# Moving expert 0's low weight parts and a weight load behind the routing, with another order of the attention rounds

## The chip, the cores and the metric

The kernel runs on one core of a Trainium2 chip. The metric is the device time of one execution in microseconds. The core has five engines with a queue each: TensorE (PE, matmuls; its weight loads are listed as PEld), VectorE (DVE), ScalarE (ACT), GpSimd (POOL) and SyncE (SP, which here only issues transfers). Each runs its own list of instructions in order, and they wait for each other by semaphores. Transfers run on 16 DMA engines; SP, ACT and POOL issue them.

## The reference

Three stages in a row, all in float32:

```
attention, for each batch (2) and head (8), state 48 x 48, 768 steps:
    y[t]  = r[t] @ (state + outer(u * k[t], v[t]))
    state = w * state + outer(k[t], v[t])
mixture of experts, on x = y with heads side by side (384 wide), 8 experts:
    fresh = argmax(x @ w_gate);  gate = sigmoid(x @ w_local)
    e[s]  = fresh[s] if s == 0 or gate[s] < 0.5 else e[s-1]
    out   = softmax(x @ w_gate)[e] * (relu(x @ w1[e]) @ w2[e])
last layer:  out = x + relu(norm(x) * g @ w_ch1) @ w_ch2
```

The expert of a token can be that of the token before it, so the choice is a scan along the sequence. The weights are w1 384 x 1024 and w2 1024 x 384 for each expert, and 384 x 1536 and 1536 x 384 for the last layer.

## The kernel before

**Attention.** The 1536 tokens are 12 chunks of 128 (NT = 12, the two batches in turn). A loop of rounds i = 0 to 13 runs on every engine, each with its own part. In round i PE makes the scores of chunk i (L1128), transposes the finished X rows of chunk i-2 (L1135), multiplies the state (L1147) and the masked scores (L1153) for chunk i-1, makes the router's logits of chunk i-2 (L1166), the state's update (L1177), and turns y back (L1184). DVE adds the diagonal term into X for chunk i-2 (L836), masks the scores (L846), sums the state (L853), scales the keys of chunk i+1 (L825) and makes the diagonal (L863, L865). ACT copies the transposed X for the router (L620), multiplies the diagonal by v, four heads before and four behind its copy of y (L609, L629), and copies the logits to LG (L632). POOL makes the products r * k (L535), the scaled r and k (L525, L544) and the decayed state (L552).

**Routing** is done in two phases: chunks 0 to 7 while the last rounds still run, and chunks 8 to 11 behind them. In each: `choose` (DVE, L762 to L771) takes the argmax and makes a code, `code_rows` (PE) turns the codes into a row, `carry_on` (DVE, L777 and L778) makes a mask of tokens that keep the expert of the one before and scans, `expert_columns` (PE) turns back, `chosen` (DVE) makes the one-hot and the gate weight, `counts` (PE) sums over tokens, and `places` (DVE, L808 to L818) gives each token its row in a buffer `xsort` in memory, sorted by expert. POOL then scatters the rows of one chunk with each indirect transfer (L518), eight for phase 0 and four for phase 1. From the counts DVE makes a small integer table `meta` (L879 to L900); each engine then loads loop bounds from it, one count at a time (`expert_regs`, L310; on SP L447 and L448).

**Weights.** Matmuls are made nearly exact by splitting each weight into a high and a low part. ACT makes the high part (`split_hi`, L359), DVE and POOL the low part by a subtraction (`split_lo`, L364), in 6 pieces of 128x1024 for each expert: POOL the first two, DVE the other four. For expert 0 this is done inside the attention rounds: ACT in rounds 6 to 11, POOL in 10 and 11, DVE in 9, 11, 12 and 13 (`LATE_LO`). There are two raw buffers. The weights of expert 2 go where those of expert 0 were; SP loads them when expert 0's are split (L417, L418, run as L342 and L344). For later experts ACT loads those of e+2 at the start of expert e's first tile.

**Experts.** Tokens of one expert are taken in tiles of 256. The first tile's rows come by one load when all scatters have landed (L433). PE transposes them (L1199), ACT and DVE round them (L654, L910), and PE multiplies, three matmuls for one product (L1204 to L1206). The rows of later tiles go by SP into a ring in X (L443), then by POOL's copy (L569) to where PE transposes them, in the middle of the tile before. PE waits at the start of each expert for all of its split pieces (`split_done`).

Of the kernel before, what the change touches and what calls it, by code (L numbers as in the profile page):

```python
# [28 lines left out]
P = 128  # L29
# [5 lines left out]
def program(nc, rkT, rows_kr, rows_v, w, u, w_small, wexp, wch, gain_in, out, xsort, ysort, dims):  # L35
# [30 lines left out]
    with ctx:  # L66
# [55 lines left out]
        M_TILES, M_BEFORE, M_ROWS, M_ENDS, M_GROUP = (i * E for i in range(5))  # L122
        M_BEHIND = M_GROUP + NG
        M_MORE = M_BEHIND + 1
        meta = sb("meta", [1, M_MORE + 1], I32)

# [125 lines left out]
        s_row = sem("code_row_made")  # L252
        s_er = sem("expert_row_made")
# [44 lines left out]
        ROUTED = (NT - 2, NT + 1)  # L298
        HALF_WEIGHTS = (2, 4, 6, 8)
        LATE_LO = (NT - 3, NT - 1, NT, NT + 1)  # L300
        def need(eng, s, n):
            if n > 0:
                eng.wait_ge(s, n)

        def expert_regs(eng, offsets=False):
# [8 lines left out]
            rows = [eng.value_load(meta[0:1, M_ROWS + e:M_ROWS + e + 1], min_val=0, max_val=TOK)  # L314
                    for e in range(E)] if offsets else None
            behind = eng.value_load(meta[0:1, M_BEHIND:M_BEHIND + 1], min_val=0, max_val=NT + E)
            more = eng.value_load(meta[0:1, M_MORE:M_MORE + 1], min_val=0, max_val=NT)
            return tiles, before, rows, behind, more
# [61 lines left out]
        def _(sp):  # L380
# [36 lines left out]
            split_done(sp, 0)  # L417
            load_weights(sp, 2)  # L418

# [14 lines left out]
            sp.wait_ge(s_meta, 1)  # L434

# [9 lines left out]

            for e in range(E):
                tiles = sp.value_load(meta[0:1, M_TILES + e:M_TILES + e + 1], min_val=1, max_val=NT)  # L447
                before = sp.value_load(meta[0:1, M_BEFORE + e:M_BEFORE + e + 1], min_val=0, max_val=NT + E)  # L448
                with sp.Fori(0, tiles) as i:
                    load_rows(before + i, nc.s_assert_within(  # L450
                        i * MT + e * CAP, e * CAP, e * CAP + TOK,
                        skip_runtime_bounds_check_because="an expert's tiles begin before its rows end"))
# [3 lines left out]
            groups = [sp.value_load(meta[0:1, M_GROUP + g:M_GROUP + g + 1], min_val=1, max_val=NT + E)  # L456
                      for g in range(NG)]
# [10 lines left out]
        def _(pool):  # L468
# [60 lines left out]
            for i in range(NT + 2):  # L529
# [25 lines left out]
                if NT - B <= i < NT:  # L555
                    split_lo(pool, 0, i - NT + B)
            assert B == POOL_CK

            for ph in range(NPH):
                scatter(ph)  # L560
# [168 lines left out]
        def _(dve):  # L729
# [101 lines left out]
            for i in range(NT + 2):  # L831
# [16 lines left out]
                if i == ROUTED[0] + 2:  # L848
                    places(0)
# [496 lines left out]
```

## Time and profile before

| | us |
|---|---|
| median of 3 runs | 416.61 (416.61, 416.61, 418.36) |
| the profiled execution | 418.34 |
| its span, first to last instruction | 416.7 |
| PE busy in the span | 375.9 (90%) |
| DVE, ACT, POOL busy | 218.6, 146.6, 138.4 |

Times in the rows are counted from the start of the span. [...]

### The profile page before, as it was taken

The numbers are of one execution on the slowest core, as the hardware profiler recorded it, in microseconds if no ns is written. First come the engines' busy times: TensorE is split into PE (matmuls) and PEld (weight loads), VectorE is DVE, ScalarE is ACT, GpSimd is POOL, SyncE is SP. The second block draws the span as 40 slices with busy tenths as digits, with TensorE's granted clock in tenths as the row PEclk, the third lists the DMA queues.
The fourth block names the chain that finished last, engine by engine and source line by source line (L and its number), as shares of the span: only waits on it lengthen the run. The fifth ranks groups of instructions, "written<-read, shape, count | busy, mean of one in ns | idle before, by whom it ended". The sixth has DMA issues, their size and how long they took to land.

```text
span 416.7 us, 7567 instructions
## 1 busy us (share of the span) xinstructions
PE 375.9 (90%) x2768; PEld 347.8 (83%) x2768; DVE 218.6 (52%) x412; ACT 146.6 (35%) x295; POOL 138.4 (33%) x134
## 2 busy tenths in 40 slices
PE   6799998660299999999999998999999999999993
PEld 5688886550299999999999997889998899988993
DVE  5687779846036647366482798675213651133110
ACT  0355676520053725438264471632002220023000
POOL 5989777384050532605235040400110000100010
PEclk9699999855589999999999999999999999999998
DMA  6989980049446774948627340600110001100000
GB/s 204 327 324 400 371 295 2 0 161 386 140 152 205 294 283 149 375 160 328 252 90 265 106 164 2 191 0 2 38 39 0 1 2 38 39 0 2 19 24 35
DMA packets 17018, 61.07 MB, mean 147 GB/s; under 512 B 2128, under 2 KB 9808, under 8 KB 14672
## 3 DMA queue, kind: packets, MB, share of 16 engines
q1 hardware_dynamic: 12240, 25.87, 17.8%
q10 hardware_dynamic: 2304, 26.74, 17.4%
q0 software_dynamic: 2432, 7.92, 5.0%
q8 instruction: 24, 0.39, 0.4%
q14 instruction: 18, 0.15, 0.1%
HBM read 49.42 MB, written 11.10 MB: 145 GB/s over the span
## 4 chain that ended last, share of the span: by engine, by line
PE 79%; DVE 8%; DMA 4%; POOL 4%; issue 3%; ACT 1%; SPq 1%; DVEq 0%; ACTq 0%; POOLq 0%
PE bank L1204 22%; PE bank L1206 22%; PE bank L1205 22%; POOL xsort L518 3%; PE bank L1128 3%; PE bank L1147 2%; PE bank L1153 2%; DMA tin<-in_rkT 2%; PE bank L1199 1%; DVE split L364 1%; PE bank L1166 1%; DMA xsort<-X,cpos 1%; PE bank L1135 1%; PE bank L1184 1%; PE bank L1177 1%
## 5 line engine op out<-in xcount | busy, mean ns | idle before, releaser
L359 ACT CAST split<-raw 128x1024 fp32r<-128x1024 f32 (+1 forms) x60 | 59.2, 1005 | 0.0
L1204 PE MATMUL bank<-xT,split 128*128 128x256 f32 x192 | 55.2, 288 | 2.1 <-DVE xT L910 2.1
L599 POOL DMA_INDIRECT out<-orow,cpos x12 | 11.6, 970 | 132.7 <-DVE orow L1039 132.7
L1205 PE MATMUL bank<-xT,split 128*128 128x256 f32 x192 | 55.0, 286 | 0.0
L1206 PE MATMUL bank<-xT,split 128*128 128x256 f32 x192 | 55.0, 286 | 0.0
L364 DVE TENSOR_TENSOR split<-raw,split 128x1024 fp32r<-128x1024 f32 (+1 forms) x40 | 51.2, 1294 | 1.9 <-ACT split L359 1.7
L1204 PE MATMUL bank<-split,h2T 128*128 128x384 f32 x144 | 48.7, 338 | 0.0
L1206 PE MATMUL bank<-split,h2T 128*128 128x384 f32 x144 | 48.2, 335 | 0.0
L1205 PE MATMUL bank<-split,h2T 128*128 128x384 f32 x144 | 48.2, 335 | 0.0
L364 POOL TENSOR_TENSOR split<-raw,split 128x1024 fp32r<-128x1024 f32 (+1 forms) x20 | 45.7, 2304 | 6.3 <-ACT split L359 6.2
L718 ACT ACTIVATE h2T<-bank 128x512 fp32r<-128x512 f32 x36 | 21.5, 598 | 72.8 <-PE bank L1206 71.7
L1051 DVE SCALAR_TENSOR_TENSOR h2T<-bank,h2T 128x512 fp32r<-128x512 f32 x36 | 24.9, 691 | 37.5 <-ACT h2T L718 37.4
L1204 PE MATMUL bank<-split,hT 128*128 128x384 f32 x128 | 43.7, 341 | 0.0
L1204 PE MATMUL bank<-split 128*128 128x512 f32 x108 | 42.1, 390 | 1.2 <-DVE split L942 1.2
L1206 PE MATMUL bank<-split,hT 128*128 128x384 f32 x128 | 42.8, 335 | 0.0
L676 ACT ACTIVATE hT<-bank 128x512 fp32r<-128x512 f32 x32 | 19.1, 597 | 67.4 <-PE bank L1206 67.4
L1205 PE MATMUL bank<-split,hT 128*128 128x384 f32 x128 | 42.8, 334 | 0.0
L1206 PE MATMUL bank<-split 128*128 128x512 f32 x108 | 42.1, 389 | 0.0
L1205 PE MATMUL bank<-split 128*128 128x512 f32 x108 | 42.1, 389 | 0.0
L958 DVE SCALAR_TENSOR_TENSOR hT<-bank,hT 128x512 fp32r<-128x512 f32 x32 | 22.0, 687 | 36.6 <-ACT hT L676 36.6
L1204 PEld LDWEIGHTS bank<-xT,split 128*128 128x128 f32 x192 | 37.6, 196 | 2.5 <-DVE xT L910 2.5
L1205 PEld LDWEIGHTS bank<-xT,split 128*128 128x128 f32 x192 | 37.6, 196 | 0.0
(161 smaller groups left out, 698.9 us busy)
## 6 DMA issues: line engine op xcount, KB each, us to landing
raw<-in_wexp ACTq DMA_DIRECT2D x14, 1536.0 KB, 9.4
tin<-in_rkT SPq DMA_DIRECT2D x12, 512.0 KB, 7.7
kr<-in_rows_kr SPq DMA_DIRECT2D x12, 384.0 KB, 6.2
raw<-in_wch ACTq DMA_DIRECT2D x2, 2304.0 KB, 9.6
xsort<-zeros SPq DMA_DIRECT2D x8, 388.0 KB, 5.3
X<-xsort SPq DMA_DIRECT2D x8, 388.0 KB, 5.9
ysort<-yrow POOLq DMA_DIRECT2D x8, 388.0 KB, 7.3
raw<-in_wexp SPq DMA_DIRECT2D x2, 1536.0 KB, 9.5
```

The lines of the kernel that those rows point to most:

```text
L359: act.copy(hi, src).then_inc(s_hi, 1)
L364: eng.tensor_tensor(lo, src, hi.bitcast(F32), ALU.subtract).then_inc(s_lop if c < POOL_CK else s_lod, 1)
L518: pool.indirect_dma_start(out=xsort, out_offset=bass.IndirectOffsetOnAxis(ap=cpos[:, j:j + 1], axis=0), in_=X[:, j, :], in_offset=None).th ...
L599: pool.indirect_dma_start(out=out, out_offset=bass.IndirectOffsetOnAxis(ap=cpos[:, j:j + 1], axis=0), in_=orow[j % 2][:, :], in_offset=Non ...
L676: act.activation(hT[:, 0, x * FU:(x + 1) * FU, :], bank[HB[x]][:].rearrange("p (f t) -> p f t", f=FU), ACT.Relu).then_inc(m_h, 1)
L718: act.activation(h2T[:, f, 0, :], bank[HB2[f % 3]][:], ACT.Relu).then_inc(f_ra, 1)
L958: dve.scalar_tensor_tensor(out=hT[:, 1, q, :].rearrange("p f t -> p (f t)"), in0=bank[HB[x]][:], scalar=0.0, in1=hT[:, 0, q, :].rearrange( ...
L1051: dve.scalar_tensor_tensor(out=h2T[:, f, 1, :], in0=bank[HB2[f % 3]][:], scalar=0.0, in1=h2T[:, f, 0, :].bitcast(F32), op0=ALU.max, op1=AL ...
L1128: last = pe.matmul(bank[2 + h][:, n * P:(n + 1) * P], kT[b][q, n, :], rT[i % 3][q, n, :], start=True, stop=True)
L1204: pe.matmul(dst, stationary[0], moving[0], start=first, stop=False)
L1205: pe.matmul(dst, stationary[0], moving[1], start=False, stop=False)
L1206: return pe.matmul(dst, stationary[1], moving[0], start=False, stop=last)
```

## The change

Five edits. The low parts of expert 0's weights leave the rounds: POOL makes its two behind the last scatter, DVE its four behind `meta`; ACT makes the high parts one round earlier (5 to 10). The load of expert 2's weights leaves SP and is done by ACT at expert 0's first tile. In a round DVE masks the scores behind the state's sum and the keys' scaling, and ACT multiplies all eight heads by the diagonal ahead of its copy for the router. In the routing of phase 0 the steps move: `choose` to the end of round 10, `code_rows` and `carry_on` to round 11, `expert_columns` to the start of round 12, `counts` to the start of round 13, `places` behind the rounds; the mask `keep` of phase 0 is made by ACT as relu(1 - code), into a new semaphore. The exponentials of phase 0 move from round 10 to 11. And each engine loads the counts that it needs in one or two instructions in place of one for each.

```diff
-        ROUTED = (NT - 2, NT + 1)
-        LATE_LO = (NT - 3, NT - 1, NT, NT + 1)
+        ROUTED = NT - 2
+        def load_many(eng, a, b, most):
+            return nc.values_load_multi_w_load_instructions(
+                meta[0:1, a:b], engines=(eng.engine,), min_val=0, max_val=most, ...)[1]
@@ expert_regs
-            tiles = [eng.value_load(meta[0:1, M_TILES + e:M_TILES + e + 1], min_val=1, max_val=NT) for e in range(E)]
+            said = load_many(eng, M_TILES, M_BEHIND + 1, NT + E)
...
+            rows = load_many(eng, M_ROWS, M_ROWS + E, TOK) if offsets else None
@@ SP
-            split_done(sp, 0)
-            load_weights(sp, 2)
...
-            sp.wait_ge(s_meta, 1)
             sp.sem_inc(m_in, 16)
...
+            tiles, before, _, _, _ = expert_regs(sp)
             for e in range(E):
-                tiles = sp.value_load(meta[0:1, M_TILES + e:M_TILES + e + 1], min_val=1, max_val=NT)
-                before = sp.value_load(meta[0:1, M_BEFORE + e:M_BEFORE + e + 1], min_val=0, max_val=NT + E)
@@ POOL
-                if NT - B <= i < NT:
-                    split_lo(pool, 0, i - NT + B)
             for ph in range(NPH):
                 scatter(ph)
+            for c in range(POOL_CK):
+                split_lo(pool, 0, c)
@@ ACT
-                if i >= 2:
-                    act.wait_ge(s_xt, i - 1)
-                    act.copy(xTa[:], bank[7][:, 0:D]).then_inc(s_xc, 1)
...
-                    dg_times_v(j, range(H // 2))
+                    dg_times_v(j).then_inc(s_dvp, 1)
+                if i >= 2:
+                    act.wait_ge(s_xt, i - 1)
+                    act.copy(xTa[:], bank[7][:, 0:D]).then_inc(s_xc, 1)
...
-                if NT - CK <= i < NT:
-                    split_hi(act, 0, i - NT + CK)
+                if NT - CK - 1 <= i < NT - 1:
+                    split_hi(act, 0, i - NT + CK + 1)
+                if i == ROUTED + 1:
+                    act.wait_ge(s_row, 1)
+                    n = PHASES[0][1] // B * P
+                    act.activation(keep[:, 0:n], bank[6][0:B, 0:n], ACT.Relu, bias=goes_on[0][0:B, 0, 1:2], scale=-1.0).then_inc(s_keep, 1)
+                    exps(0)
+            exps(1)
...
-                    if starts and e > 0:
+                    if starts:
                         split_done(act, e)
                         load_weights(act, e + 2)
@@ DVE
@@ carry_on
+                if ph == 0:
+                    dve.wait_ge(s_keep, 1)
+                else:
+                    link(dve.tensor_scalar(keep[:, a:b], bank[6][0:B, 0:b - a], 0.0, None, ALU.is_equal))
@@ the rounds: in round i now X, stsum, scale_k(i + 1), masks sc, rku, dg, and then
-                if i == ROUTED[0]:
+                if i == ROUTED:
+                    dve.wait_ge(s_late, 1)
+                    choose(0)
+                if i == ROUTED + 1:
                     carry_on(0)
-                if i == ROUTED[0] + 1:
+                if i == ROUTED + 2:
                     chosen(0)
-                if i in LATE_LO:
-                    split_lo(dve, 0, POOL_CK + LATE_LO.index(i))
+            places(0)
...
+            for c in range(POOL_CK, CK):
+                split_lo(dve, 0, c)
             dve.sem_inc(m_y, XR)
@@ PE
+                if i == ROUTED + 2:
+                    expert_columns(0)
+                if i == ROUTED + 3:
+                    counts(0)
                 if i >= 2:
                     pe.wait_ge(s_x, i - 1)
...
-                if i == ROUTED[0] + 2:
-                    counts(0)
...
-                if i == ROUTED[0]:
+                if i == ROUTED + 1:
                     pe.wait_ge(s_late, 1)
                     code_rows(0)
-                if i == ROUTED[0] + 1:
-                    expert_columns(0)
```

## Rows read from the trace of the kernel before

**Rows 1.** The chain that ended last, by engine (the page).

```profile
PE 79%; DVE 8%; DMA 4%; POOL 4%; issue 3%; ACT 1%; SPq 1%; DVEq 0%; ACTq 0%; POOLq 0%
```

**Rows 2.** Stretches: length, busy of PE, PEld, DVE, ACT, POOL, PEclk, DMA, GB/s.

```profile
64.01:69.60 5.59, 5.59 (x80) 4.68 (x80) 5.45 (x14) 3.66 (x12) 3.05 (x3) 1.00 0.00 0
...
80.50:113.20 32.70, 11.78 (x69) 9.07 (x69) 13.65 (x61) 4.78 (x16) 13.59 (x12) 0.50 0.62 219
113.20:116.80 3.60, 3.60 (x17) 3.60 (x18) 0.00 (x0) 0.00 (x0) 0.00 (x0) 0.50 0.18 32
```

**Rows 3.** The chain in order of time: start, us, what.

```profile
101.56 4.91 DMA xsort<-X,cpos
106.53 2.98 DMA xrow<-xsort
```

**Rows 4.** Timeline of POOL, scatters 1, 4, 9, 12: start, us, engine, what, [idle before].

```profile
83.51 2.08 POOL L518 DMA_INDIRECT xsort<-X,cpos  x1 [5.95 <-DVEq L819]
...
88.42 1.91 POOL L518 DMA_INDIRECT xsort<-X,cpos  x1 [0.30 <-issue]
...
97.77 0.96 POOL L518 DMA_INDIRECT xsort<-X,cpos  x1 [2.37 <-DVEq L819]
...
101.56 0.96 POOL L518 DMA_INDIRECT xsort<-X,cpos  x1 [0.30 <-issue]
```

**Rows 5.** Timeline of ACT in round 9.

```profile
60.15 0.48 ACT L620 COPY xTa<-bank 128x384 f32<-128x384 f32 x1 [0.75 <-PE bank L1135]
60.52 1.01 ACT L609 ACTIVATE dv<-vn,dg 128x48 f32<-128x48 f32 x4
```

**Rows 6.** Timeline of DVE beside the scatters.

```profile
83.31 1.23 DVE L364 TENSOR_TENSOR split<-raw,split 128x1024 fp32r<-128x1024 f32 x1
...
88.28 1.22 DVE L364 TENSOR_TENSOR split<-raw,split 128x1024 fp32r<-128x1024 f32 x1
...
97.27 0.17 DVE L818 CAST cpos<-ec 128x4 int32<-128x4 f32 x1
...
101.61 0.14 DVE L896 CAST meta<-cnt 1x1 int32<-1x1 f32 x1
```

**Rows 7.** Timeline, one POOL and one DVE product side by side, and the latter alone.

```profile
61.31 0.97 POOL L552 TENSOR_TENSOR state<-stsum,wst 128x192 f32<-128x192 f32 x1 [1.10 <-DVE stsum L853]
61.75 0.95 DVE L863 TENSOR_TENSOR rku<-rk,ub 128x384 f32<-128x384 f32 x1
...
74.25 0.55 DVE L863 TENSOR_TENSOR rku<-rk,ub 128x384 f32<-128x384 f32 x1
```

**Rows 8.** Timeline of PE and DVE from round 11 on, the waits of the routing.

```profile
70.90 1.21 DVE L778 TENSOR_TENSOR_SCAN er<-keep,bank 2x512 bf16<-2x512 f32 x1
...
72.94 0.55 PE L1135 MATMUL bank<-ident,X 128*128 128x128 f32 x3 [1.85 <-DVE X L836]
...
80.46 0.90 PE L1135 MATMUL bank<-ident,X 128*128 128x128 f32 x3 [3.52 <-DVE X L836]
...
87.81 0.56 DVE L836 TENSOR_TENSOR X<-bank,dv 128x384 f32<-128x384 f32 x1 [3.27 <-ACT dv L609]
...
91.58 0.18 DVE L762 TENSOR_REDUCE mx<-LG 128x4 f32<-128x32 f32 x1 [2.08 <-ACT LG L632]
```

**Rows 9.** DMA issues near 86, 115 and 151.7: KB each, median us to landing.

```profile
xsort<-X,cpos POOLq DMA_INDIRECT x2, 3.3
...
X<-xsort SPq DMA_DIRECT2D x1, 388.0 KB, 3.3
...
X<-xsort SPq DMA_DIRECT2D x1, 388.0 KB, 8.4
```

**Rows 10.** Timeline of POOL and PE, tile 2's rows in the first tile.

```profile
118.63 0.83 POOL L569 COPY xrow<-X 128x768 f32 x1 [16.11 <-DMA X<-xsort]
...
123.52 0.82 PE L1199 MATMUL bank<-ident,xrow 128*128 128x128 f32 x6
```

**Rows 11.** SP's loads of single counts: duration ns min/median/max.

```profile
L447 SPq TENSOR_LOAD <-meta x8: 262/266/275, 107.0 to 179.0; - x8
```

More of the change, by code:

```diff
@@ L118, in program @@
         cnt_i = sb("cnt_i", [1, 2, E], I32)
[L122 to L125, printed above, removed]
+        M_TILES, M_MORE, M_BEHIND, M_GROUP = 0, E, E + 1, E + 2
+        M_ROWS, M_ENDS = 2 * E, 3 * E
+        assert M_GROUP + NG <= M_ROWS
+        meta = sb("meta", [1, M_ENDS + E], I32)
         gcol = sb("gcol", [P, KD])
@@ L303, in need @@
                 eng.wait_ge(s, n)
+        def load_many(eng, a, b, most):
+            return nc.values_load_multi_w_load_instructions(
+                meta[0:1, a:b], engines=(eng.engine,), min_val=0, max_val=most,
+                skip_runtime_bounds_check_because="counts of rows that there are, and of their tiles")[1]
         def expert_regs(eng, offsets=False):
             eng.wait_ge(s_meta, 1)
-            tiles = [eng.value_load(meta[0:1, M_TILES + e:M_TILES + e + 1], min_val=1, max_val=NT) for e in range(E)]
+            said = load_many(eng, M_TILES, M_BEHIND + 1, NT + E)
+            tiles = [nc.s_assert_within(said[e], 1, NT, skip_runtime_bounds_check_because="counts rounded up to tiles, "
+                                        "at least one") for e in range(E)]
+            more = nc.s_assert_within(said[M_MORE], 0, NT, skip_runtime_bounds_check_because="one less than a number of tiles")
             before = [0]
@@ L313, in expert_regs @@
                 before.append(eng.snap(before[e] + tiles[e], min_val=0, max_val=NT + E))
[L314 to L318, printed above, removed]
+            rows = load_many(eng, M_ROWS, M_ROWS + E, TOK) if offsets else None
+            return tiles, before, rows, said[M_BEHIND], more
         def over_tiles(eng, e, tiles, more, tile):
@@ L444, in load_rows @@
                              xsort[bass.ds(start, MT), :].rearrange("(h p) d -> p h d", p=P)).then_inc(m_in, 16)
+            tiles, before, _, _, _ = expert_regs(sp)
             for e in range(E):
[L447 to L450 removed]
+                with sp.Fori(0, tiles[e]) as i:
+                    load_rows(before[e] + i, nc.s_assert_within(
                         i * MT + e * CAP, e * CAP, e * CAP + TOK,
@@ L455, in _ @@
                     sp.wait_ge(s_fill, 16 * (e + 2))
-            groups = [sp.value_load(meta[0:1, M_GROUP + g:M_GROUP + g + 1], min_val=1, max_val=NT + E)
-                      for g in range(NG)]
+            groups = [nc.s_assert_within(x, 1, NT + E, skip_runtime_bounds_check_because="a group's rows are of one expert at least")
+                      for x in load_many(sp, M_GROUP, M_GROUP + NG, NT + E)]
             for g in range(NG):
@@ L605, in _, with dg_times_v, exps @@
         def _(act):
-            def dg_times_v(j, heads):
+            def dg_times_v(j):
                 b = j % B
-                for h in heads:
+                for h in range(H):
                     last = act.activation(dv[b][:, h, :], vn[j % VRING][:, h, :], ACT.Copy, scale=dg[b][:, h:h + 1])
                 return last
+            def exps(ph):
+                act.wait_ge(s_sub, ph + 1)
+                act.activation(pe_[:, slice(*PHASES[ph])], le[:, slice(*PHASES[ph])], ACT.Exp).then_inc(s_exp, 1)
             for i in range(NT + 2):
@@ L857, in _ @@
                 if i < NT:
+                    b = i % B
+                    dve.wait_ge(s_scp, i + 1)
+                    need(dve, s_yp, i - B + 1)
+                    for h in range(2):
+                        dve.tensor_tensor(sc[b][:, h], bank[2 + h][:].rearrange("p (n t) -> p n t", n=NP),
+                                          causal[:].unsqueeze(1).broadcast_to([P, NP, P]), ALU.mult).then_inc(s_sc, 1)
                     dve.wait_ge(s_rk, i + 1)
```

26 lines of the change are left out of this document (3 added, 23 removed).

## The prediction

> **What bounds the kernel.** I read the chain of waits by engine first [rows 1]: TensorE (PE) carries 79% of the span, so a change beside PE pays only where PE waits. The table by stage says where that is [rows 2]: an attention round in full swing (64.0 to 69.6) keeps PE busy for all of its 5.59 us at the full clock, while from 80.5 to 113.2 it works 11.8 of 32.7 us, at half clock. Last I read what ends that gap [rows 3]: the last of 12 row scatters (issued at 101.56, landed 4.91 us later at 106.47), then the load of the sorted rows (2.98 us), then 6.65 us of transposes, register work and rounding to the first expert product at 113.2. Everything before the change's stage is bound by PE, everything behind 113.2 by PE too; the change lives in the stretch between 64 and 113, and there the chain is: places of phase 0, eight scatters, places of phase 1, four scatters, landing. The scatters themselves leave every 1.27 us (97.77 to 101.56 is three of them) [rows 4].
>
> **The parts.**
>
> *Attention rounds.* VectorE (DVE) does the state sum and the key scaling ahead of the masks, ScalarE (ACT) does all eight diagonal products ahead of the copy for the router. Nothing is added, and PE fills the whole round [rows 2], so I cost it at nothing. What hides it: ACT waits 0.75 us for PE before its copy, and four diagonal products take it 1.01 [rows 5]; the second four now stand in front too, so the copy comes about 0.3 late, and PE reads it only behind two groups of 16 matmuls. If the diagonal came late, every round would pay (a rival below).
>
> *The low parts leave rounds 9 to 13.* DVE gives up four subtractions of 1.23 us [rows 6] and GpSimd (POOL) two. DVE and POOL also block each other: POOL's state product at 61.31 takes 0.97, the DVE product begun meanwhile at 61.75 takes 0.95, and the same product with POOL quiet at 74.25 takes 0.55 [rows 7]. So the X additions of rounds 11 and 12, for which PE waited 1.85 and 3.52 us [rows 8], come earlier. But on that same path the change puts the carry mask on ACT, behind its logits copy. Step by step: round 11 starts on PE at 69.6; scores, transposes, both products and the code row end at about 73.5; ACT is free for the mask only behind PE's logits, 74.5, and needs about 0.6; DVE's scan takes 1.21 [rows 8], so the expert row is there at 76.3. PE stands still from 74.9 to 76.4, now in front of round 12. Round 12 has 45 of round 10's 80 matmuls, the longer ones, about 3.7 us at full clock, plus 0.6 for the ACT copy in its middle: 81.0. Before, the counts were done 0.9 us after 80.46 and the places 1.9 us later (a subtraction starts behind them at 83.31) [rows 6, 8]. Now counts at 81.2, the last X addition to 81.5, places done at 83.2. **The first scatter stays at 83.5.** That is my main reading: phase 0 gains nothing, because its counts and places now stand behind round 12's work.
>
> *Phase 1 comes 8 us earlier.* Its first instruction waited for the last logits until 91.58, held up by half-clock PE work, a 3.27 us wait of DVE for the diagonal products at 87.81, and one more subtraction [rows 8]. Now the logits follow the X addition at 81.5 by about 2.1 us: 83.6. Its own work took 5.86 us (91.58 to 97.44) [rows 6, 8], so its places are ready at 89.5 and the counts table (4.3 us, 97.44 to 101.75) at 93.8. Before, POOL had run dry for 2.37 us in front of scatter 9 [rows 4], of which 0.3 is the usual gap. That 2.07 us goes: the 12 scatters now run in one row. What is late next is POOL's issuing itself.
>
> *The subtractions land on the scatters.* Scatters 1 and 4 took 2.08 and 1.91 us against 0.96 for the others, and each starts within 0.2 us of a DVE subtraction (83.31, 88.28) [rows 4, 6]: each waited until that ended. DVE now runs its four subtractions from 93.8 to 98.4, on top of scatters 9 to 12. If POOL slips in between two of them, as its state product did [rows 7], each hit scatter waits about 1.0 and its successor starts inside the next but one subtraction: two are hit, 2.0 us, the same as the 2.07 lost before. If none is hit: 0. If POOL stays shut out for all four: 4.6. I take 2.0. The sum for the last scatter's issue: 83.5 + 11 x 1.27 + 2.0 = 99.5, against 101.56: 2.1 us earlier. POOL's two own subtractions then end at about 105.2 and the first product needs them at about 109: hidden, with 4 us to spare.
>
> [...] The rows show long scatters beside a DVE tensor-tensor subtraction [rows 4, 6]. [...]
>
> *The third weight load leaves the window.* Two transfers of 1536 KB started at 89.6; scatters that were issued before them landed after 3.3 us, the last one, in their wake, after 4.91 [rows 3, 9]. With nothing beside it I take 3.0, as the rows' own load took [rows 3]; the ends are 3.3, and 2.7 if half a neighbour's issue was in that: 1.9 us earlier. It is issued now by ACT at the start of the first expert tile (about 112.3 in the old times). Price there: a row load without weights beside it lands in 3.3 us, with them in 8.4 [rows 9]. The rows of tile 2 would land near 121 to 122.5 and POOL's 0.83 us copy end at 122 to 123.4, against 119.5 before; PE reads them at 123.52 [rows 10]. So the cover shrinks from 4 us to about nothing. POOL's subtractions for expert 1 slip 3 us behind the copy and push DVE's. I take 0.6 us of PE waiting at the first tile and its border, from 0 to 3.
>
> *One load for the counts.* On SyncE (SP) a count costs a 0.27 us load and about 0.3 of checks [rows 11]; two per expert go, ten in one instruction come once, between 0.3 and 2.7 us, behind the issue of the first row load, and hide or cost under the previous point. I take 0. On the other engines the loads ran in the wait for the rows, and they start 8 us earlier now.
>
> *Clock.* PE restarts cold behind the gap either way: 3.6 us at half clock behind 113.2 [rows 2], which cost 1.8. Another such stretch may come out longer or not; I take 0.3, from 0 to 1.8.
>
> **Sum**: 2.1 + 1.9 - 0.6 - 0.3 = 3.1 us faster. The profiled execution took 418.34 (416.7 of span, 1.6 around it), which is 1.7 above the median; the difference carries over: 415.2 for an execution like that one, **413.5** for the median.
>
> **Rivals.**
> [...]
> - *POOL is shut out by four subtractions in a row*: last issue at 102.0, 2.6 later than forecast, 416.1. Against: [rows 7].
> - *PE falls to half clock in front of round 12.* It fell before in the 3.52 us wait and did not in the 1.85 us one [rows 2, 8]; the new wait is 1.5 plus a short one behind it. If it falls, the 3.7 us of round 12 take 3 more, all places come 3 us later, last issue 102.5: 416.5.
> - *Slower: the router's copy misses PE in every round.* ACT's eight diagonal products (two times 1.01 us) need the diagonal, which DVE now makes behind the masks, and both stand in front of the copy. In the old times PE wants the copy about 7.5 us after the previous masks begin. It decides where the diagonal is ready more than 1.2 us later than I reckon (DVE held by POOL's key product in each round). At 0.7 a round over ten rounds: 7.0 - 3.1 slower, 420.5. For: DVE and POOL hold each other up already. Against: PE's full round, and DVE's idle share.
> - That the change does nothing can be only if the end of the gap is set elsewhere; the chain [rows 3] leaves no other.
>
> **Numbers.** Forecast 0.55, no hold-up 0.12, shut out 0.11, half clock 0.12, slower 0.10. Half a per cent, 2.1 us, is about what can be told from no change: faster means under 414.5. Of the forecast's 0.55 about 0.47 lies below that, with 0.12 from the first rival: faster 0.59; same 0.31 (0.08 + 0.11 + 0.12); slower 0.10. The forecast's own range is 411.8 to 415.3; for 8 in 10 it must hold the two cases near 416 and most of the first rival: 411.0 to 417.0.
>
> **What would show it.** Right: first scatter near 83.5, no gap in front of the ninth, the last issued near 99.5 and landing in about 3; scatters 9 to 12 alternately 0.96 and 2; first expert product near 109.2; a PE wait below 1 us in the first tile. Wrong: PE waits inside rounds 3 to 9; half clock before 82; a first scatter beyond 85; all four last scatters long; a wait of more than 2 us for the rows of the second tile.

## The result, and the profile after

The changed kernel took 419.0 us (median of 20 runs, 416.6 to 421.51), the kernel before, run beside it, 417.99 (20 runs, 416.19 to 418.92): a ratio of 1.0042, 95% interval 1.0026 to 1.0057. It is 0.4% slower. 413.5 was forecast, 411.0 to 417.0 the range, so the time lies outside it. Part of the distance is the base: 413.5 was counted down from a median of three runs, 416.61, and the median of 20 is 417.99; from that one the same sum gives 414.9. Ratios here leave out runs more than 1.5% above the fastest of their kernel: three of 12 with the load issued later, one of 12 with the start repaired, and none of the others. The profiled execution took 421.01 with a span of 419.2, at the upper end of its runs; the one of before had 416.7. The two traces differ by 2.5 us of span, and the rows say where.

The chain by engine has hardly changed its shape [rows 1]; this is its line:

```profile
PE 80%; DMA 6%; DVE 5%; issue 3%; POOL 3%; SPq 1%; ACT 1%; POOLq 0%; DVEq 0%
```

The table by stretches of the kernel after (window, us of it, then busy time of PE, PEld, DVE, ACT and POOL, the granted clock PEclk as a share of full speed, the DMA share, GB/s) answers to [rows 2]:

```profile
64.84:70.39 5.55, 5.55 (x79) 4.64 (x78) 4.97 (x14) 3.88 (x14) 1.93 (x2) 1.00 0.00 0
75.50:77.50 2.00, 0.35 (x6) 0.16 (x4) 1.43 (x3) 2.00 (x9) 0.00 (x0) 1.00 0.00 0
77.50:78.00 0.50, 0.01 (x1) 0.00 (x0) 0.50 (x2) 0.34 (x2) 0.00 (x0) 0.54 0.00 0
78.00:83.00 5.00, 4.97 (x37) 3.82 (x38) 1.33 (x9) 0.75 (x2) 0.00 (x0) 0.50 0.00 0
...
113.41:118.00 4.59, 4.59 (x21) 4.59 (x22) 0.00 (x0) 0.34 (x1) 0.00 (x0) 0.50 0.79 284
118.00:118.50 0.50, 0.50 (x5) 0.50 (x4) 0.21 (x1) 0.50 (x2) 0.00 (x0) 0.50 0.95 399
118.50:119.00 0.50, 0.50 (x6) 0.50 (x6) 0.48 (x1) 0.50 (x1) 0.00 (x0) 1.00 1.03 434
```

A round in full swing is as full as before. The third column from the right, the clock, matters here: PE works 0.35 of the 2 us up to 77.5, the clock falls to half, and round 12, in which PE does not stand still (4.97 of 5.00 us), runs at half clock. Behind the gap the half clock lasts from 113.41 to 118.5, 5.1 us, where it was 3.6 [rows 2].

The timeline of the same kernel (start, us, engine, line, operation, count, and in brackets the idle time before it and what ended that) shows the waits of the routing, the scatters and the first tile, against [rows 4], [rows 6], [rows 8] and [rows 10]:

```profile
75.22 0.67 ACT L640 ACTIVATE keep<-bank,goes_on 2x512 f32<-2x512 f32 x1
...
76.00 1.21 DVE L783 TENSOR_TENSOR_SCAN er<-keep,bank 2x512 bf16<-2x512 f32 x1 [2.07 <-ACT keep L640]
...
77.27 0.25 PE L1096 MATMUL bank<-identb,er 2*128 2x2 bf16 x4 [1.65 <-DVE er L783]
78.03 0.90 PE L1140 MATMUL bank<-ident,X 128*128 128x128 f32 x3 [0.52 <-DVE X L841]
...
85.05 0.56 DVE L841 TENSOR_TENSOR X<-bank,dv 128x384 f32<-128x384 f32 x1 [5.58 <-PE bank L1185]
...
87.52 1.19 POOL L517 DMA_INDIRECT xsort<-X,cpos  x1 [15.53 <-DVEq L824]
...
88.82 0.19 DVE L764 TENSOR_REDUCE mx<-LG 128x4 f32<-128x32 f32 x1 [1.65 <-ACT LG L634]
...
97.86 0.96 POOL L517 DMA_INDIRECT xsort<-X,cpos  x1 [0.30 <-issue]
...
99.10 4.68 DVE L369 TENSOR_TENSOR split<-raw,split 128x1024 fp32r<-128x1024 f32 x4
...
100.39 1.96 POOL L517 DMA_INDIRECT xsort<-X,cpos  x1 [0.30 <-issue]
102.65 1.96 POOL L517 DMA_INDIRECT xsort<-X,cpos  x1 [0.30 <-issue]
104.63 4.64 POOL L369 TENSOR_TENSOR split<-raw,split 128x1024 fp32r<-128x1024 f32 x2
...
124.81 1.08 POOL L566 COPY xrow<-X 128x768 f32 x1 [15.54 <-DMA X<-xsort]
...
125.95 0.77 PE L1200 MATMUL bank<-ident,xrow 128*128 128x128 f32 x5 [1.41 <-POOL xrow L566]
```

PE's waits of 1.85 and 3.52 us for the X additions [rows 8] have become one of 1.65 and one of 0.52, in front of round 12. What follows is long: round 12 keeps PE from 78.0 to 85.0, DVE stands idle for 5.58 us until its last X addition, and the first scatter is at 87.52 instead of 83.51. Of these 4.0 us 0.8 are older than round 12: rounds 2 to 10 all begin that much later than before (round 2 at 20.52 instead of 19.67, round 10 at 64.84 instead of 64.01). Phase 1's choice begins at 88.82 instead of 91.58, and the gap of 2.37 us in front of the ninth scatter [rows 4] is gone; the last is issued at 102.65, 1.1 later than before, of which two held-up scatters make 2.0.

The chain in order of time (start, us, what), against [rows 3] and the loads of [rows 9]:

```profile
102.65 4.02 DMA xsort<-X,cpos
106.75 0.38 SPq L435
...
114.73 9.67 DMA X<-xsort
124.84 1.06 POOL xrow L566
125.95 0.88 PE bank L1200 x6
```

The last scatter takes 4.02 us from issue to landing, 1.0 of it the hold-up, so about 3.0 with no weights beside it. The first product starts at 113.41, against 113.18 before: the later scatter and the quicker landing cancel. Then the load of the second tile's rows takes 9.67 us, and PE stands for 1.41 us in the middle of the first tile. From the start of the first tile to that of the second, 21.57 us pass instead of 19.34: those 2.2 us, and the 0.2 in front, are the whole difference of the traces.

Each run also records its span and mean granted clock. The 20 runs of the kernel after lie between (span 414.4, clock 0.954) and (419.8, 0.939), six of them at 0.938 or 0.939 with spans of 419.1 to 419.8, the profiled one among them. So the share of half clock is not the same in every run; what it costs is what the experiments had to give.

### The profile page after: what moved, and what is told of

Read it like the earlier page. It is cut to its first block, busy times and chain, and to the rows that moved or that the text cites. A ratio compares the mean times of both kernels' runs of the same rounds, so it can differ in the third digit from the quotient of the medians.

```text
span 419.2 us, 7375 instructions
## 1 busy us (share of the span) xinstructions
PE 377.9 (90%) x2768; PEld 349.8 (83%) x2768; DVE 216.0 (52%) x410; ACT 146.6 (35%) x296; POOL 136.4 (33%) x134
## 4 chain that ended last, share of the span: by engine, by line
PE 80%; DMA 6%; DVE 5%; issue 3%; POOL 3%; SPq 1%; ACT 1%; POOLq 0%; DVEq 0%
PE bank L1205 21%; PE bank L1206 21%; PE bank L1207 21%; PE bank L1156 3%; PE bank L1150 3%; PE bank L1129 3%; POOL xsort L517 2%; DMA X<-xsort 2%; PE bank L1167 2%; PE bank L1185 2%; DMA tin<-in_rkT 2%; PE bank L1140 1%; PE bank L1178 1%; PE bank L1200 1%; DMA xsort<-X,cpos 1%
## 5 line engine op out<-in xcount | busy, mean ns | idle before, releaser
L369 DVE TENSOR_TENSOR split<-raw,split 128x1024 fp32r<-128x1024 f32 (+1 forms) x40 | 52.8, 1340 | 2.1 <-ACT split L364 1.9
```

The costliest lines, as they stand in the source:

```text
L369: eng.tensor_tensor(lo, src, hi.bitcast(F32), ALU.subtract).then_inc(s_lop if c < POOL_CK else s_lod, 1)
```

## The experiments

Four theories stood against each other, and the text below calls them by these names. The clock theory: the clock that falls in the wait in front of round 12 costs what was forecast as gain. The load theory: the third weight load (that of expert 2) costs more at the first tile than it gives at the last landing. The order theory: the reordered rounds cost something that I had put at nothing. The scatter theory: the low parts on the scatters cost more than the old gap. The A and B in the recorded expectations are those of each run alone. Ratios below are to runs of the kernel before taken beside them, with the 95% interval. The filler products write to a PSUM bank that nobody reads and take nothing out of the computation.

**PE kept busy in the wait** (the kernel after, with fillers):

```diff
+                     keep_busy(24)
                      expert_columns(0)
+                     keep_busy(8)
```

`keep_busy(n)` makes n products of 128x128 in bf16; both calls stand at the start of round 12.

> The changed kernel, with 24 small matmuls on an unused PSUM bank ahead of TensorE's wait for the expert row in round 12 and 8 behind the expert columns. Theory A (the clock falls to half in the gap between 75.6 and 78.0, and round 12 pays for it): the granted clock stays 1.00 through round 12, the first scatter goes from 87.5 to 84 to 84.7, the last one leaves about 3 us earlier, and the time falls by 2.5 to 3.5 us against the changed kernel (ratio to before 0.995 to 0.998). Rival B (the first scatter is late for the order of the steps, not the clock): first scatter stays above 86.5, time unchanged at 1.004.

Measured: 415.84 us (6 runs, 415.29 to 416.71), 0.9948 (0.9932 to 0.9964), against 1.0042 without: 0.9% by the ratios, 3.2 us by the medians, for a row of products that nobody uses. The table by stretches and the timeline:

```profile
75.60:78.00 2.40, 2.09 (x35) 1.76 (x33) 2.05 (x5) 2.09 (x10) 0.00 (x0) 1.00 0.00 0
78.00:83.00 5.00, 4.39 (x50) 3.47 (x50) 2.33 (x13) 1.23 (x3) 0.00 (x0) 1.00 0.01 3
```

```profile
77.88 0.55 PE L1146 MATMUL bank<-ident,X 128*128 128x128 f32 x3
...
82.43 0.55 PE L1146 MATMUL bank<-ident,X 128*128 128x128 f32 x3 [0.59 <-DVE X L841]
...
84.30 1.18 POOL L517 DMA_INDIRECT xsort<-X,cpos  x1 [12.47 <-DVEq L824]
```

The clock stays at full up to 83.0, round 12 takes 3.9 us (77.88 to 81.8), the first scatter is at 84.30 (forecast 83.5), the last at 99.99 (99.5), the first product at 109.39 (109.2). The clock theory holds, and with the clock kept, the forecast's sum for the gap holds nearly step by step. What is left of the forecast's shortfall is behind 109: here too PE waits 1.41 us for the second tile's rows.

**The same fillers in the kernel before**, in its two waits:

```diff
+                 if i in (NT - 1, NT):
+                     keep_busy(24 if i < NT else 56)
```

> The kernel before, with filler matmuls in its two waits for X: 24 in round 11, 56 in round 12. Theory A (the clock's fall is a loss of both kernels; in the kernel before it delays phase 1, not the first scatter): clock 1.00 through round 12, first scatter unchanged near 83.5, phase 1's places 2 to 3 us earlier, so GpSimd's gap in front of scatter 9 closes and the time falls by 1.5 to 2.1 us, ratio 0.995 to 0.997. Rival B (the kernel before gains nothing since GpSimd's issuing bounds it): 1.000.

Measured: 415.95 us (12 runs), 0.9954 (0.9937 to 0.9971). The old order gained too: the ninth scatter came at 93.84, with its gap down to 0.62, and the last at 97.63, 3.9 us earlier than before. Of these 0.8 stood there from round 2 on (18.83 instead of 19.67), and the first tile gave 1.05 back (20.39 us instead of 19.34, with 6.2 us at half clock behind the gap instead of 3.6), so the span is 2.1 shorter. So with the clock held on both sides the change is worth 0.06%, nothing. The clock explains why it came out slower; it does not by itself explain why it isn't 3 us faster.

**The third weight load alone** (the kernel before, this one part done):

```diff
-             split_done(sp, 0)
-             load_weights(sp, 2)
...
-                     if starts and e > 0:
+                     if starts:
```

> The kernel before, with nothing changed but the load of expert 2's weights: no longer by SyncE when expert 0's parts are split, but by ScalarE at the first tile. Theory A: the last scatter lands 3.0 us after its issue in place of 4.9 (1.9 gained) and the second tile's rows land in 8 to 10 us in place of 3.3 (2.0 to 2.5 lost in the first tile): net between 0 and 1 us slower, ratio 1.000 to 1.003. Rival B (the load costs nothing at the tile, the loss of the changed kernel comes from its late low parts): 1.5 to 2 us faster, 0.995 to 0.997.

Measured: 417.49 us (12 runs), 0.999 (0.9974 to 1.0005). Its chain:

```profile
101.81 2.64 DMA xsort<-X,cpos
...
113.19 9.45 DMA X<-xsort
```

and PE's timeline, the first tile's transposes and the second's:

```profile
108.92 1.54 PE L1197 MATMUL bank<-ident,xrow 128*128 128x128 f32 x6 [13.34 <-issue]
...
124.84 0.88 PE L1197 MATMUL bank<-ident,xrow 128*128 128x128 f32 x6 [1.41 <-POOL xrow L567]
```

The last scatter lands after 2.64 us instead of 4.91 [rows 3]: what the prediction gained there, 1.9, is there, and 0.4 more. But only 0.6 of it reaches the first product (112.55 against 113.18). The first tile's rows, whose load was issued at 104.52 and took 3.0, lay ready at 107.5, and PE began at 108.92, released by "issue": by nothing that the profile shows. The program has only PE's register work on the counts in this place (here still the single loads), so that is the likely cause; no run has this load moved and the counts in one load, and nothing else. Then the row load of tile 2 takes 9.45 us, PE waits 1.41 for it, and the first tile takes 21.33, 2.0 more. In the timed runs gain and loss cancel. The load theory holds in the form that the part is worth nothing, and the trace shows an interplay that the prediction lacked: this part needs the counts earlier or loaded faster to be worth its 2 us in front of the first product. In the kernel after they are both, and its row load is followed by the first product after 6.66 us, as before, not 8.03.

**The load issued later** (the kernel after; expert 2's weights issued behind the rounding of the second tile's rows):

```diff
-                         load_weights(act, e + 2)
+                         if e > 0:
+                             load_weights(act, e + 2)
...
+                         if starts and e == 0:
+                             load_weights(act, 2)
```

> The changed kernel, with the load of expert 2's weights issued by ScalarE behind the rounding of the second tile's rows (about 12 us later) in place of at the start of the first tile. Theory A (the second tile's rows stand behind the weights in the DMA engines: landing 9.7 us after issue, TensorE waits for them in the first tile): the row load lands in 3 to 4 us, the wait of about 2.4 us in the first tile goes, and the kernel is 2.0 to 2.5 us faster than the changed one, so about level with the kernel before (ratio 0.998 to 1.000). Rival B (the row load is slow for another reason, the fill of zeros or the four-row prefetch): landing stays over 8 us and the time stays where the changed kernel's is, 1.004.

Measured: 417.58 us (12 runs, 414.07 to 421.44), 0.9973 (0.9941 to 1.0004). By the means of all runs this kernel is level with the one before (417.69 against 417.72) and 1.6 us under the one after (419.25). The DMA issues from 109 to 140 us (operation, count, KB each, median us to landing):

```profile
raw<-in_wexp ACTq DMA_DIRECT2D x4, 1536.0 KB, 12.4
X<-xsort SPq DMA_DIRECT2D x4, 388.0 KB, 3.3
```

The row loads land in 3.3 us again, PE waits for none of them, and the first tile takes 19.85 instead of 21.57. The weights' own 12.4 us are hidden. The wide interval is the clock again: three of these runs have 0.938 or 0.939, at 420.4 to 421.4, four 0.956 or more, at 414.1 to 414.9.

**Both repairs** (fillers and late load):

> The changed kernel with both repairs: the filler matmuls before and behind the expert columns in round 12, and expert 2's weights loaded behind the rounding of the second tile's rows. Theory A (clock and weight load are two separate losses of the changed kernel, about 3 and 2.2 us, and add up): 5 to 6 us faster than the changed kernel, 413 to 414, ratio to before 0.989 to 0.992, all runs within 2 us of each other. Rival B (one of them hides the other): no better than with the filler alone, 0.995.

Measured: 415.53 us, 0.9944 (0.9923 to 0.9964). That is the rival's figure: only 0.3 us under the fillers alone, where 1.4 was to be had. The trace names the rest: no wait for rows, but behind the gap the half clock lasted till 115.9, 6.2 us, and the first tile took 20.44; and round 2 began at 21.34, where the kernel before has 19.67. That second number pointed at the order theory.

**The start of the rounds** (the kernel after; in round 0 alone the masks stand ahead of the next round's key scaling, as before the change):

```diff
-                 if i + 1 < NT:
-                     scale_k(i + 1)
-                 if i < NT:
+                 def masks():
...
+                 if i == 0:
+                     masks()
+                 if i + 1 < NT:
+                     scale_k(i + 1)
```

> The changed kernel with one edit: in round 0 VectorE masks the scores before it scales the keys of round 1. Theory A (the new order costs about 1 us at the start, once, and every later round is shifted by it): round 2 starts at 19.0 to 19.9 in place of 20.2 to 21.3, the time falls by 0.7 to 1.5 us against the changed kernel, ratio to before 1.000 to 1.003. Rival B (the start shifts with the arrival of the transfers): ratio stays 1.004 and round 2 starts beyond 20.2.

Measured: 417.59 us (12 runs, 414.18 to 422.12), 1.0 (0.9971 to 1.0029), against 1.0042 (1.0026 to 1.0057). The timelines of the kernel after and of this one, in that order:

```profile
13.41 2.08 PE L1129 MATMUL bank<-rT,kT 64*128 64x128 f32 x16 [4.26 <-DVE sc L855]
...
10.28 1.78 DVE L830 TENSOR_TENSOR kT<-tin,wn 128x512 f32<-128x512 f32 x1 [2.42 <-DMA tin<-in_rkT]
11.99 1.28 DVE L855 TENSOR_TENSOR sc<-bank,causal 128x512 f32<-128x512 f32 x2
```

```profile
9.27 1.29 DVE L853 TENSOR_TENSOR sc<-bank,causal 128x512 f32<-128x512 f32 x2 [0.84 <-PE bank L1135]
10.48 1.74 DVE L830 TENSOR_TENSOR kT<-tin,wn 128x512 f32<-128x512 f32 x1
...
12.32 1.16 PE L1135 MATMUL bank<-rT,kT 64*128 64x128 f32 x16 [3.16 <-DVE kT L830]
```

In round 0 the key scaling waits 2.42 us for a transfer (`tin<-in_rkT`). In the changed order the masks queue behind it and PE's next scores wait for them (4.26 us). With the masks first they are done in that wait, and the scores start 1.1 us earlier, at 12.32. Once the rounds are in swing the two orders are equal: 5.54 us from round 2 to 3 and from there on, in both (20.52 to 26.06 and 18.12 to 23.66). All traces together say the same: round 1's scores start at 13.41 to 14.30 in the six with the changed order, at 12.49 to 13.14 in the four with the old one, and at 11.86 to 13.20 in the four with the masks first in round 0. The order theory holds, as a cost of the first rounds alone, about 1.1 us, and not in the form of the prediction's slower rival.

Two things in this pair are not the edit's. Round 2 starts 2.4 us earlier, not 1.1, since the clock, which fell at 13.9 here and at 12.7 in the kernel after, was back at 17.3 here and at 19.5 there. Such a stretch of half clock in round 1 lasted 3.4 us in four of the 14 traces and 6.8 in ten; the short ones are three of the four with the masks first, one of the four with the old order and none of the six with the changed one, and no run shows whether the order has a part in that. And in round 12 of this trace, which has no fillers, the clock fell as well, but came back in the middle of the round:

```profile
75.00:77.50 2.50, 1.98 (x17) 1.54 (x16) 1.92 (x10) 0.93 (x3) 0.00 (x0) 0.56 0.00 0
77.50:83.00 5.50, 4.34 (x44) 3.40 (x40) 1.86 (x8) 1.23 (x3) 0.00 (x0) 0.89 0.01 3
```

It was at half from 75.3 to 78.7. So of the 4.1 us by which the first scatter is earlier (83.44 against 87.52), the new start has 2.4 and the clock in round 12 the rest.

**The start and both repairs together:**

> As the kernel with both repairs, and VectorE masks the scores of round 0 before it scales the keys of round 1, as the kernel before does; all later rounds keep the new order. Theory A (in round 0 the masks stand behind the keys' transfer, and TensorE's second scores wait for them, which delays every round by about 0.5 us): the second scores start at 13.0 to 13.2 in place of 13.4 to 14.3, and the time falls by 0.3 to 0.8 us. Rival B (the later start comes from when the transfers arrive): no difference.

Measured: 413.6 us (412.73 to 414.92), 0.9912 (0.989 to 0.9935): 1.9 us between its median and that of both repairs alone, 0.3% by the ratios. 0.3 to 0.8 us was forecast. Rounds 1 and 2 begin at 11.86 and 17.88 instead of 14.24 and 21.34, and all of these 3.46 us are still there at the first scatter, 81.82 against 85.28. Here too a part is the clock's: in round 1 it was at half for 3.4 us instead of 6.8.

**The carry mask back on DVE** (both repairs, 16 fillers in place of 24):

```diff
-                     act.activation(keep[:, 0:n], bank[6][0:B, 0:n], ACT.Relu, bias=goes_on[0][0:B, 0, 1:2], scale=-1.0)...
...
+                 link(dve.tensor_scalar(keep[:, a:b], bank[6][0:B, 0:b - a], 0.0, None, ALU.is_equal))
```

> As the kernel with both repairs, but the mask of phase 0 is made by VectorE from the code row, as in the kernel before, with 16 filler matmuls in place of 24 since the gap is shorter. Theory A (the mask on ScalarE waits behind its logits copy and costs 0.8 to 1.0 us on the path to the expert row): expert row 0.8 to 1.0 us earlier, first scatter and total earlier by 0.7 to 0.9 us. Rival B (the last X addition and round 12 hide it): no difference in the total.

Measured: 414.23 us (413.52 to 414.91), 0.9925 (0.9906 to 0.9944), against 0.9944 (0.9923 to 0.9964) for both repairs alone. Its timeline, and then that of the kernel with ACT's mask:

```profile
74.90 0.68 DVE L779 TENSOR_SCALAR keep<-bank 2x512 f32<-2x512 f32 x1 [0.46 <-PE bank L1084]
75.62 1.21 DVE L780 TENSOR_TENSOR_SCAN er<-keep,bank 2x512 bf16<-2x512 f32 x1
```

```profile
75.99 0.17 ACT L634 COPY LG<-bank 128x9 f32<-128x9 f32 x1 [0.48 <-PE bank L1176]
76.06 0.67 ACT L640 ACTIVATE keep<-bank,goes_on 2x512 f32<-2x512 f32 x1
...
76.83 1.21 DVE L786 TENSOR_TENSOR_SCAN er<-keep,bank 2x512 bf16<-2x512 f32 x1 [2.06 <-ACT keep L640]
```

The same mask takes 0.68 us on DVE, which stood idle at that point, and 0.67 on ACT, where it queues behind a logits copy that needs PE's products. The scan and the first scatter (85.28 against 84.07) both come 1.2 us later with ACT's mask, but 0.3 of that was there when round 11 began (71.22 against 70.89): the mask's place costs 0.9 us on the path, as expected. In the timed runs it is 0.2%, within intervals that overlap.

**The low parts back in the rounds** (the kernel after, this part undone):

```diff
+                 if NT - B <= i < NT:
+                     split_lo(pool, 0, i - NT + B)
...
+                 if i in (NT - 3, NT - 1, NT, NT + 1):
+                     split_lo(dve, 0, ...)
```

> The changed kernel, with expert 0's low parts back in the rounds (VectorE in 9, 11, 12, 13, GpSimd in 10, 11); order of the rounds, late weight load and single loads of the counts stay. Theory A (moving the low parts costs 2.0 us on the last two scatters and gives back the time in the rounds): scatters 11 and 12 take 0.96 us, but the first scatter is later by 1 to 2 us since TensorE waits longer around round 11 and 12; time within 1 us of the changed kernel. Rival B (the low parts on the scatters are what made it slow): 2 us faster than the changed kernel, ratio to before 0.999.

Measured: 420.46 us (6 runs), 1.0052 (1.0035 to 1.0069). The timeline of DVE and POOL:

```profile
78.06 1.23 DVE L369 TENSOR_TENSOR split<-raw,split 128x1024 fp32r<-128x1024 f32 x1
79.20 0.55 DVE L841 TENSOR_TENSOR X<-bank,dv 128x384 f32<-128x384 f32 x1
...
87.30 1.22 DVE L369 TENSOR_TENSOR split<-raw,split 128x1024 fp32r<-128x1024 f32 x1
...
90.43 1.18 POOL L517 DMA_INDIRECT xsort<-X,cpos  x1 [15.12 <-DVEq L824]
...
104.55 0.96 POOL L517 DMA_INDIRECT xsort<-X,cpos  x1 [0.30 <-issue]
```

One subtraction sits in front of an X addition, one in front of the places, and the first scatter is at 90.43, 2.9 later; all twelve scatters take 0.96 or (the first) 1.18, for no subtraction runs beside them, and 2.0 of it comes back, half by the last issue (104.55 against 102.65) and half in the last scatter itself: the first product starts 0.8 us later (114.24 against 113.41). The scatter theory falls: moving the low parts is a small gain or nothing (the intervals overlap).

**The counts in one load** (the kernel before, this part alone: one load of ten numbers on each engine in place of single ones, a second of eight where the rows' counts are needed, the layout of the counts changed to suit it):

> The kernel before with one edit of the change: the counts read in one or two loads on each engine. Theory A (these loads run in the wait for the rows and cost and bring nothing but about 1 us between SyncE's row loads, which nothing waits for): ratio 0.999 to 1.001. Rival B (they shorten the way to the first product): 1 us faster, 0.997 to 0.998.

Measured: 418.29 us (12 runs), 1.0014 (0.9991 to 1.0038). No effect that can be told, in the place where it was put: in the trace the first product stands 6.64 us behind the issue of the row load (105.93 to 112.57), 6.65 in the kernel before, and PE's transposes wait for the rows in both. Behind an earlier landing they may show, as the kernel with the weight load alone suggests.

**All repairs:** start, fillers, mask on DVE, and the third weight load behind the second activation of the first tile:

> All repairs together: filler matmuls, the mask of phase 0 on VectorE, masks first in round 0, and expert 2's weights loaded in the middle of the first tile. Theory A (four separate losses of 3, 0.9, 1 and 2 us, of which the clock's ramp behind the gap takes some back at random): 412 to 413, ratio to before 0.987 to 0.990. Rival B (their gains overlap): no better than the best of them, 0.991 to 0.993.

Measured: 412.83 us (412.28 to 415.49), 0.9911 (0.9881 to 0.9941). First product at 107.32, first tile 19.10 us. By the ratio this is the rival's case, no better than the start and both repairs (0.9912): the gain of the mask can't be told. Round 2 began at 19.76 here, with 6.8 us of half clock around round 1, against 17.88 and 3.4 there, so that part of the start's gain was not in this trace.

**And two of the four low parts of DVE moved** into its wait in round 12:

```diff
+                     for c in (POOL_CK, POOL_CK + 1):
+                         split_lo(dve, 0, c)
...
-             for c in range(POOL_CK, CK):
+             for c in range(POOL_CK + 2, CK):
```

> As the kernel with all repairs, and two of VectorE's four low parts moved from behind the counts into its wait of round 12, behind the one-hot of phase 0. Theory A (each low part beside a scatter can hold it up by 1 us, and POOL slips in between two, so two low parts hit one scatter where four hit two): one long scatter, last issue 0.7 to 1.0 us earlier than in the kernel with all repairs if the last X addition is not pushed out; it costs up to 0.5 if it is. Rival B (the long scatters have another cause): two long scatters as before.

Measured: 411.63 us (5 runs, 410.54 to 412.13), 0.9859 (0.9834 to 0.9884). Its timeline:

```profile
77.21 2.35 DVE L369 TENSOR_TENSOR split<-raw,split 128x1024 fp32r<-128x1024 f32 x2
...
92.79 2.36 DVE L369 TENSOR_TENSOR split<-raw,split 128x1024 fp32r<-128x1024 f32 x2
...
93.87 0.98 POOL L517 DMA_INDIRECT xsort<-X,cpos  x1 [0.30 <-issue]
...
96.42 0.96 POOL L517 DMA_INDIRECT xsort<-X,cpos  x1 [0.30 <-issue]
```

One long scatter was expected, two by the rival; none is held up. The last is issued at 96.42 instead of 97.96, of which 0.5 is in the first scatter already (82.27 against 82.80), and the first product starts at 105.95 instead of 107.32. This kernel is faster than both kernels of the change: 1.4% under the one before, where the change as made lost 0.4%. Against all repairs alone the intervals touch (0.9884 and 0.9881).

## Why the prediction was wrong

**The step that failed is "PE stands still from 74.9 to 76.4 [...] Round 12 has 45 of round 10's 80 matmuls, the longer ones, about 3.7 us at full clock", and on it "The first scatter stays at 83.5".** The wait was as long as worked out (1.65 us and 0.52), but in the profiled run the clock fell in it, and round 12 took 7.0 us; the first scatter came 4.0 late, 0.8 of it from the start. With fillers the round takes 3.9 us and the scatter is at 84.3. The price is 0.9% of the kernel's time, 3.9 us (1.0042 less 0.9948), or 3.2 by the medians. I had this as a rival at 0.12, argued from a wait of 3.52 us after which the clock was half and one of 1.85 after which it was not [rows 8]. Two waits in one execution don't say what a third will do. Three traces have this wait and no fillers, a fourth has a longer one (1.65 and 1.65, low parts back), and the clock fell in or behind it in all four: at 77.5, 1.9 us after PE's last work (the kernel after); at 79.1, 1.3 us into round 12 (load issued later); at 75.3 (start); at 78.9 (low parts back). Round 12 took 7.0, 5.9, 5.3 and 7.0 us by that. With fillers no run of seven kernels had a mean clock below 0.950; without them the kernel after had 0.938 or 0.939 in six runs and 0.954 in one. The rival should have had a chance above a half.

**"I take 0.6 us of PE waiting at the first tile and its border, from 0 to 3"** was too little: the wait is 1.41 us, in the kernel after, with the load moved alone, and with fillers. The working had it: rows at 121 to 122.5, the copy's end at 122 to 123.4, PE at 123.52. The trace of after has the load issued at 114.73 (121 to 122.5 less 8.4 is 112.6 to 114.1), 9.67 us instead of 8.4 [rows 9], and the copy 1.08 instead of 0.83 [rows 10]. Three terms at the edge of the cover, each a little over. The other side of the edit, 1.9 us at the last scatter's landing, was right (2.3 with the load moved alone). The forecast counted this part at +1.3; the part alone measured nothing (0.999, 0.9974 to 1.0005).

**"Clock [...] I take 0.3, from 0 to 1.8".** Behind the gap PE ran 5.1 us at half clock instead of 3.6, which is 0.75 us of work. Together with the 1.41 this is 2.16 of the 2.23 us by which the first tile was longer. The half clock there lasted from 3.1 to 6.2 us among these kernels' traces, with the same work in it, and the first tile follows it: about 17.5 us plus half of that stretch plus the wait for rows, where there is one (before 17.5 + 1.8 = 19.3, measured 19.34; with all repairs 17.5 + 1.55 = 19.05, measured 19.10). That is scatter on every number of this section.

**"PE fills the whole round, so I cost it at nothing"** held for the rounds in swing and not for the first ones, where PE doesn't fill the round and DVE waits for a transfer. I read round 10 and took it for all. Masks first in round 0 give 1.0 against 1.0042 in one pair and 0.9912 against 0.9944 in the other: 0.4% and 0.3%, 1.3 to 1.8 us, each with intervals that overlap a little. The later start of about 1.1 us is shown in the traces; the price in the time is likely, not fixed closer, and the repaired start is slightly ahead of the old one (round 1's scores start at 12.5 on average, against 12.85 in the old order and 14.0 in the changed one): of these 1.45 us 1.1 are a loss against the kernel before.

**The mask on ACT** was worked out right (expert row at 76.3 forecast, 77.2 measured, with round 11 beginning 0.8 later) but taken as given; it is 0.9 us on the path that ACT's mask alone puts there.

**A slip that the sum does not use:** "then 6.65 us of transposes, register work and rounding" counts from the issue of the row load at 106.53 and holds its 2.98 us; behind the rows' landing it is 3.7 us to the first product at 113.2.

**What was right:** the gap in front of the ninth scatter went; the last scatters were held up by 1.0 us each, two in the kernel after, at the predicted size of 2.0. In the eight kernels that keep the four subtractions there, the hold-up is 1.0 (four of them), 1.55 (two) or 2.0 (two), as the two rows happen to meet; with two subtractions it was 0, with none 0. The "no hold-up" of the prediction's numbers (there also "the first rival", 0.12) is the case that scatters 9 to 12 take 0.96 us each beside DVE's four subtractions, 2.0 us better than the forecast. It did not come in any of these eight: in the kernel after the last two took 1.96 each, and with the low parts back in the rounds, where no subtraction runs beside them, those four took 0.96. By what a subtraction holds a scatter up, no run shows. POOL's own subtractions were hidden (104.63 to 109.27, the first product at 113.41), the counts in one load moved nothing by itself, and the prediction's slower rival, the router's copy missing PE in every round, did not happen: rounds of 5.55 us.

**The balance**, against the sum of 3.1: with fillers the kernel is 0.9948 of the one before, 2.2 us faster. Its trace has the first product 3.8 us earlier (forecast 4.0) and gives 2.05 back in the first tile (forecast 0.9). Without fillers 3.9 more go, which makes the kernel 1.8 slower (1.0042). What stays open: why the clock falls earlier or later behind the same wait, and why it came back 3.4 us later in one trace and stayed at half through the round in the three others. No experiment varied that wait alone, and the runs of one kernel differ in nothing that I set.

## What to carry to other kernels

A wait that moves from behind an engine's last full stretch to a place in front of one was not neutral on TensorE here: round 12 behind it took 7.0 us, with the clock held by fillers 3.9. Look at what follows such a wait, and price that at half clock with a good chance (it fell in four traces of four here); cheap products on an unused bank in the wait were worth 0.9% here, in the old order 0.5%. When a large load leaves one critical transfer, find the transfer that it now meets and add up its cover term by term; a cover of "about nothing" was a wait of 1.41 us here. And a reordered loop is to be read in its first round too, where other things can be late than in the tenth: here PE waited 4.26 us for the masks in front of round 1, where round 10 kept it busy for all of its 5.55 us.

## What the runs showed of the hardware

- The row load of 388 KB for the second tile landed in 3.1 to 3.3 us in the nine traces with no weight transfer issued in the 10 us before it, and in 8.98 to 9.67 in the five where two of 1536 KB had been issued 2.3 to 3.0 us before it on another queue.
- Where a row load was issued 0.4 to 1.7 us ahead of these two (five traces), it landed in 3.0 to 3.5 us and they in 7.2 to 13.2; issued 0.02 us ahead of them (carry mask back on DVE), it landed in 9.8.
- The spread of a kernel's runs is itself a reading: 419.0 had 4.9 us between the ends of its 20 runs, the same kernel with fillers 1.4 between those of 6, and in the list of runs span and clock go together, from 414.4 us at 0.954 to 419.8 at 0.939.
- Two DVE subtractions of 1.2 us in a row beside the scatters held up none of them (one trace), four held up one or two, by 1.0 to 2.0 us together (eight traces).
- In all 14 traces the clock was at half around round 1, for 3.4 us in four and 6.8 in ten. The round took 5.8 to 6.0 us in the four and 5.9 to 7.1 in the ten; round 2 took 5.54 to 5.56 us in all 14.
